# Whole 128x128 transposes with copies by parity, sinks ahead of transposes and reciprocals ahead of masks, in a banded attention on one core

## What is computed

```python
scores = scale * np.matmul(q, k.transpose(0, 1, 3, 2))
keep = is_sink | in_window
scores = np.where(keep, scores, -1000000000.0)
a = np.exp(scores - np.max(scores, axis=-1, keepdims=True))
a = a / (np.sum(a, axis=-1, keepdims=True) + 1e-09)
x = np.matmul(a, v)                       # heads side by side: 1536 x 512
x = np.maximum(x @ w_in, 0.0) ** 2 @ w_out          # 512 -> 2048 -> 512
h = x @ w2_in                                        # 512 -> 1024
solu = h * softmax(h)
out = (solu - mean) / sqrt(var + 1e-06) * g_ln @ w2_out
```

## Time and profile before

| | |
|---|---|
| median of 3 runs | 499.36 us (498.99 to 499.49) |
| profiled execution | 499.36 us, span of its profile 497.6 us |
| TensorE busy | 481.1 us, 97% of the span |
| VectorE, ScalarE, GpSimd busy | 58%, 50%, 21% |
| exponentials L480 | 46.7 us in 96 |
| scaling L402 | 45.7 us in 48 |
| DMA | 25.97 MB, nearly all in the first 130 us |

### The profile page before, as it was taken

How to read it: one execution, slowest core, us unless ns; L and a number is a source line. 1 busy time by engine, 2 the same in 40 slices (tenths; PEclk the granted TensorE clock), 3 DMA queues, 4 the chain that set the end, 5 groups by cost and what they waited for, 6 DMA issues and landing times.

```text
span 497.6 us, 7811 instructions
## 1 busy us (share of the span) xinstructions
PE 481.1 (97%) x2742; PEld 387.4 (78%) x2742; DVE 287.4 (58%) x678; ACT 248.0 (50%) x539; POOL 106.7 (21%) x129
## 2 busy tenths in 40 slices
PE   6889897999999999999999999999999999999997
PEld 3656575787888888888888888888888888888885
DVE  5788776368677454334435433444497666666651
ACT  3978878433443453344345334434356555545441
POOL 1876666049998000000000000000000000000000
PEclk9999999999999999999999999999999999999999
DMA  6768821170000000000000000000000000000001
GB/s 199 290 238 308 316 98 36 44 297 0 0 0 0 0 1 1 0 0 0 0 1 0 0 1 0 0 0 1 0 1 22 22 21 21 21 21 21 21 28 57
DMA packets 10138, 25.97 MB, mean 52 GB/s; under 512 B 3200, under 2 KB 5248, under 8 KB 8832
## 3 DMA queue, kind: packets, MB, share of 16 engines
q1 hardware_dynamic: 10112, 25.64, 14.1%
HBM read 22.48 MB, written 3.15 MB: 52 GB/s over the span
## 4 chain that ended last, share of the span: by engine, by line
PE 86%; ACT 6%; DVE 3%; DMA 3%; SPq 1%; POOL 1%; issue 1%; DVEq 0%
PE ps L1023 26%; PE ps L1038 26%; PE ps L1073 13%; PE ps L1052 13%; ACT probs L480 3%; PE ps L1059 2%; DMA k_sb<-in_k_t 2%; PE ps L951 2%; PE ps L906 1%; PE ps L915 1%; PE ps L961 1%; ACT pt_sb L488 1%; SPq L320 1%; POOL probs L402 1%; ACT x_hi L494 1%
## 5 line engine op out<-in xcount | busy, mean ns | idle before, releaser
L790 DVE CAST act_hi<-act_sq 128x512 fp32r<-128x512 f32 x48 | 26.0, 542 | 126.1 <-ACT act_sq L538 123.3
L533 ACT ACTIVATE ps<-ps 128x512 f32<-128x512 f32 x48 | 27.9, 582 | 141.4 <-PE ps L1023 141.4
L1023 PE MATMUL ps<-x_hi,w_in_hi 128*128 128x512 f32 x192 | 75.1, 391 | 0.0
L1038 PE MATMUL ps<-act_hi,w_out_hi 128*128 128x512 f32 x192 | 74.8, 390 | 0.1
L1023 PE MATMUL ps<-x_hi,w_in_lo 128*128 128x512 f32 x192 | 74.8, 389 | 0.0
L1023 PE MATMUL ps<-x_lo,w_in_hi 128*128 128x512 f32 x192 | 74.7, 389 | 0.0
L1038 PE MATMUL ps<-act_hi,w_out_lo 128*128 128x512 f32 x192 | 74.7, 389 | 0.0
L1038 PE MATMUL ps<-act_lo,w_out_hi 128*128 128x512 f32 x192 | 74.7, 389 | 0.0
L402 POOL TENSOR_TENSOR probs<-probs,row_inv 128x512 f32<-128x512 f32 (+1 forms) x48 | 45.7, 973 | 30.8 <-DVE row_inv L691 30.8
L480 ACT ACTIVATE probs<-probs,neg_max 128x272 f32<-128x272 f32 (+2 forms) x96 | 46.7, 497 | 7.1 <-DVE neg_max L678 7.0
L1023 PEld LDWEIGHTS ps<-x_hi,w_in_hi 128*128 128x128 f32 x192 | 36.0, 188 | 8.5 <-issue 1.2
(11 more groups left out here) (97 smaller groups left out, 829.3 us busy)
## 6 DMA issues: line engine op xcount, KB each, us to landing
w_in_raw<-in_w_in SPq DMA_DIRECT2D x4, 1024.0 KB, 4.8
w_out_raw<-in_w_out SPq DMA_DIRECT2D x4, 1024.0 KB, 8.2
k_sb<-in_k_t SPq DMA_DIRECT2D x8, 408.0 KB, 5.1
q_sb<-in_q_t SPq DMA_DIRECT2D x8, 384.0 KB, 4.2
v_sb<-in_v SPq DMA_DIRECT2D x16, 192.0 KB, 3.9
out<-out_sb SPq DMA_DIRECT2D x12, 256.0 KB, 2.0
w_in_raw<-in_w_in SPq DMA_DIRECT2D x1, 2048.0 KB, 9.4
w_out_raw<-in_w_out SPq DMA_DIRECT2D x1, 2048.0 KB, 13.8
```

Source lines behind the costliest of these rows:

```text
L533: nc.scalar.activation(ps[:, H_BANK + u, :], ps[:, H_BANK + u, :], ACT.Relu).then_inc(relu_done, 1)
L790: dve.tensor_copy(act_hi[:, u, :], act_sq[:, u, :]).then_inc(act_hi_done, 1)
L1023: last = mm(ps[:, H_BANK + u, :], w[:, u, c, :], x[:, c, t * TILE1:(t + 1) * TILE1], start=(c == 0 and m == 0), stop=(c == DC - 1 and m == 2))
L1038: last = mm(ps[:, Y_BANK + c, :], w[:, u, c * P:(c + 1) * P], a[:, u, :], start=(first and m == 0), stop=(final and m == 2), skip_group_ch ...
```

## The change

The numbered pieces of the diff: (1) each block is turned by one 128x128 transpose; a unit fills one bank, unit n bank 4 + n % 2. (2) ScalarE copies the even units, VectorE the odd ones; a unit waits for the copy of unit n-2 alone, and `weigh_key` for the copy of its own unit. (3) In step 0 of pair p keys 4, 5 and the sinks of pair p-1 stand ahead of the transposes. (4) The sinks take one 128-column matmul for both heads in place of two of 64 columns. (5) VectorE's `invert` stands ahead of `mask_group` in each step.

```diff
--- before.py
+++ after.py
@@ -188,15 +189,6 @@
     gen_ps = ps[:, S_BANK:S_BANK + 2, :].rearrange("p a b -> p (a b)")[:, 0:SEQ]
     gen_pt_ps = ps[:, PT_BANK:PT_BANK + 2, :].rearrange("p a b -> p (a b)")[:, 0:SEQ]
 
-    HQ = P // 2
-
-    def turned_part(m, h):
-
-        chunks = 8 if m < NG - 1 else 7
-        src = ps[:, PT_BANK + h, 0:HQ * chunks].rearrange("p (g q) -> p g q", q=HQ)
-        dst = pt_sb[:, :, :].rearrange("p n (g h q) -> p (n g) h q", g=4, h=2)[:, 8 * m:8 * m + chunks, h, :]
-        return dst, src
-
     def score_bank(g, u):
 
         return S_BANK + 2 * u + g % 2
...
@@ -481,11 +473,10 @@
                                                         bias=neg_max[:, b, u, i:i + 1], accum_out=row_sum[:, b, u, i:i + 1])
                 last.then_inc(exp_done, 1)
 
-            def copy_turned(p, m):
-
-                act.wait_ge(turned, NG * p + m + 1)
-                dst, src = turned_part(m, 0)
-                nc.scalar.activation(dst, src, ACT.Copy).then_inc(pt_low, 1)
+            def copy_turned(p, n):
+
+                act.wait_ge(turned, UNITS * p + n + 1)
+                nc.scalar.activation(pt_sb[:, n, :], ps[:, PT_BANK + n % 2, :], ACT.Copy).then_inc(pt_even, 1)
 
             def x_high(p):
 
...
@@ -500,7 +491,7 @@
                     for m in range(NG):
                         if m == 0 and p > 0:
                             x_high(p - 1)
-                        copy_turned(p, m)
+                        copy_turned(p, 2 * m)
                         if p < LAST:
                             exps(p + 1, m)
                     if p == 0:
...
@@ -690,11 +681,11 @@
                 dve.wait_ge(den_done, NG * p + k + 1)
                 dve.reciprocal(row_inv[:, b, :, blocks], row_den[:, b, :, blocks]).then_inc(inv_done, 1)
 
-            def copy_turned(p, m):
-
-                dve.wait_ge(turned, NG * p + m + 1)
-                dst, src = turned_part(m, 1)
-                dve.tensor_copy(dst, src).then_inc(pt_high, 1)
+            def copy_turned(p, n):
+
+                dve.wait_ge(turned, UNITS * p + n + 1)
+                width = 512 if n < QB - 1 else 3 * P
+                dve.tensor_copy(pt_sb[:, n, 0:width], ps[:, PT_BANK + n % 2, 0:width]).then_inc(pt_odd, 1)
 
             def x_low(p):
 
...
@@ -711,13 +702,13 @@
                 invert(0, 1)
                 for p in range(PAIRS):
                     for m in range(NG):
-                        if p < LAST:
-                            mask_group(p + 1, m)
                         if m == 0:
                             invert(p, 2)
                         elif p < LAST:
                             invert(p + 1, m - 1)
-                        copy_turned(p, m)
+                        if p < LAST:
+                            mask_group(p + 1, m)
+                        copy_turned(p, 2 * m + 1)
                         if m == 0 and p > 0:
                             x_low(p - 1)
                     if p == 0:
...
@@ -907,31 +898,25 @@
                                       keys[:, key:key + BAND_WIDTH[i]], start=True, stop=True)
                     last.then_inc(scores_done, 1)
 
-            def turn(n, g, columns):
-
-                for h in range(2):
-                    half = slice(HQ * h, HQ * (h + 1))
-                    at = 4 * HQ * (n % 2) + HQ * g
-                    last = nc.tensor.transpose(ps[:, PT_BANK + h, at:at + HQ], columns[half, :], identity[half, half])
-                return last
-
-            def turn_units(p, m):
-
-                b = p % 2
-                macro = NG * p + m
-                wait(pe, pt_low, macro)
-                wait(pe, pt_high, macro)
-                for n in (2 * m, 2 * m + 1):
-                    pe.wait_ge(probs_ready, (QB + 1) * p + min(n + 2, QB))
-                    for u in range(2):
-                        if n < QB - 1:
-                            turn(n, 2 * u, probs[:, b, u, own_at(n):own_at(n) + P])
-                            last = turn(n, 2 * u + 1, probs[:, b, u, prev_at(n + 1):prev_at(n + 1) + P])
-                        else:
-                            turn(n, u, probs[:, b, u, own_at(n):own_at(n) + P])
-                if m == NG - 1:
+            def turn(p, u, n, to, src):
+
+                at = to + (2 * P * u if n < QB - 1 else P * u)
+                return nc.tensor.transpose(ps[:, PT_BANK + n % 2, at:at + P], probs[:, p % 2, u, src:src + P], identity[:, :])
+
+            def turn_unit(p, n):
+
+                unit = UNITS * p + n
+                pe.wait_ge(probs_ready, (QB + 1) * p + min(n + 2, QB))
+                if unit >= 2:
+                    pe.wait_ge(pt_even if n % 2 == 0 else pt_odd, unit // 2)
+                for u in range(2):
+                    last = turn(p, u, n, 0, own_at(n))
+                    if n < QB - 1:
+                        last = turn(p, u, n, P, prev_at(n + 1))
+                if n == QB - 1:
                     pe.wait_ge(probs_ready, (QB + 1) * (p + 1))
-                    last = turn(QB - 1, 2, sink_probs[:, b, :, :, :].rearrange("p u i s -> p (u i s)"))
+                    sinks = sink_probs[:, p % 2, :, :, :].rearrange("p u i s -> p (u i s)")
+                    last = nc.tensor.transpose(ps[:, PT_BANK + n % 2, 2 * P:3 * P], sinks, identity[:, :])
                 last.then_inc(turned, 1)
 
             def weigh_key(p, j):
...
@@ -940,8 +925,7 @@
                 if j == 0:
                     pe.wait_ge(v_in[b], 16 * V_LOADS * (p // 2 + 1))
                     wait(pe, x_lo_done, 2 * p)
-                pe.wait_ge(pt_low, NG * p + j // 2 + 1)
-                pe.wait_ge(pt_high, NG * p + j // 2 + 1)
+                pe.wait_ge(pt_even if j % 2 == 0 else pt_odd, 3 * p + j // 2 + 1)
 
                 width = 2 * P if j < QB - 1 else P
                 cuts = [(0, P), (P, P)] if j == 2 else [(0, width)]
...
@@ -956,10 +940,8 @@
 
                 for i in range(2, QB):
                     col = P * i
-                    for u in range(2):
-                        rows = slice(HEAD_DIM * u, HEAD_DIM * (u + 1))
-                        last = mm(ps[rows, X_BANK + col // HALF, col % HALF:col % HALF + P], v_sinks[:, p % 2, i - 2, rows],
-                                  pt_sb[:, QB - 1, 2 * P:3 * P], start=False, stop=True, skip_group_check=True)
+                    last = mm(ps[:, X_BANK + col // HALF, col % HALF:col % HALF + P], v_sinks[:, p % 2, i - 2, :],
+                              pt_sb[:, QB - 1, 2 * P:3 * P], start=False, stop=True, skip_group_check=True)
                 last.then_inc(pv_done, 1)
 
             def banded_attention():
...
@@ -968,11 +950,12 @@
                 score_group(1, 0)
                 for p in range(PAIRS):
                     for m in range(NG):
-                        turn_units(p, m)
                         if m == 0 and p > 0:
                             weigh_key(p - 1, 4)
                             weigh_key(p - 1, 5)
                             weigh_sinks(p - 1)
+                        turn_unit(p, 2 * m)
+                        turn_unit(p, 2 * m + 1)
                         if m > 0:
                             weigh_key(p, 2 * m - 2)
                             weigh_key(p, 2 * m - 1)
```

More of the change, by code:

```diff
@@ L20 @@
 NP, NG = len(PIECES), len(GROUPS)
+UNITS = QB
 BAND_WIDTH = [P, 2 * P] + LATE * [BAND]
@@ L95, in build @@
     probs = att.take("probs", [P, 2, 2, ALL_BANDS])
-    pt_sb = att.take("pt_sb", [P, QB, 512])
+    pt_sb = att.take("pt_sb", [P, UNITS, 512])
     probs_end = att.at
@@ L226, in build @@
     turned = sem("turned")
-    pt_low = sem("pt_low_copied")
-    pt_high = sem("pt_high_copied")
+    pt_even = sem("pt_even_copied")
+    pt_odd = sem("pt_odd_copied")
     pv_done = sem("pv_done")
```

## The result

The changed kernel takes 505.12 us (median of 4 runs, 504.92 to 505.44), the kernel before 499.43 us beside it: the ratio is 1.0113, 95% interval 1.0101 to 1.0126. It is 5.7 us slower; forecast were 4.3 us, 503.7 in 501.2 to 506.9.

A forecast was written before the change was run, and what follows sets the result against it. A loop through ScalarE, VectorE, GpSimd and TensorE was taken to bound each attention pair. Middle pairs +2.1 us, first interval +0.5, pair 0 +1.0, last interval +0.7: together +4.3 on 499.36, so 503.7 us, range 501.2 to 506.9.

The forecast's parts named there:

- main term: Five middle pairs of the banded attention: 5 x 10.04 = 50.2 us against 48.06, +2.1.
- the ends: Attention before and after the five middle pairs: pair 0 +1.0 us, first interval +0.5, last interval +0.7.
- Part 4, the wait of VectorE: Sums and reciprocals ahead of the masks: VectorE waits for exponentials, and ScalarE idles 0.7 us, twice a pair.
- Part 2, transposes: Whole transposes on TensorE at 0.110 us a step: 23 blocks x 0.044 = 1.0 us more a pair.
- The new loop: One pair from x_hi through exponentials, reciprocal, masks, scores, transposes, values and sinks to the next x_hi: 10.04 us.
- The two are a tie: taking either cause away alone frees little.: Per pair, TensorE's queue without waits takes 9.97 us, the loop by way of VectorE 10.04; removing one cause frees little.
- TensorE's own round: TensorE's own queue over one pair, with no wait at all: 9.97 us.
- second rival: Gain of the earlier sinks cancels the rest: a pair 9.5 us, total 499.7; chance 0.07.
- Part 1: Sinks and values of pair p-1 ahead of pair p's transposes: up to 0.95 us a pair off ScalarE's wait of 1.33.
- The faster rival: ScalarE is freed before x_hi and the rest hides: a pair 8.8 us, total 495.8; chance 0.06.
- The k_sb waits: TensorE's two waits for k_sb in the middle pairs, 0.6 us each, vanish in the slower loop.
- Rival D: Waits for x_hi, masks and unit 5's copy add, or whole-shape changes cost 0.3: a pair 10.6 us, 507.5; chance 0.13.

The follow-up runs named there:

- e_split: The changed kernel with the sums and reciprocals of steps 1 and 2 between the masks of the group's first and second block; 499.96 us, ratio 1.0023.
- e_whole_sinks: The changed kernel with the reciprocals behind the masks again; 499.74 us, ratio 1.0011 to the kernel before.
- e_sinks_recip: The kernel before with keys 4, 5 and sinks ahead of the half transposes and reciprocals ahead of the masks; 506.26 us, ratio 1.0146.
- S: Keys 4, 5 and sinks of pair p-1 ahead of the transposes; alone on the kernel before 496.46 us, ratio 0.9942.
- e_sinks_wide: The kernel before with keys 4, 5 and sinks ahead of the half transposes, and sinks as 4 matmuls of 128 columns; 497.22 us.
- e_best: The kernel before with sinks ahead of the half transposes and VectorE's copy ahead of the reciprocals in steps 1 and 2; 496.34 us, repeated 495.80.

## Why the prediction was right, point by point

- **Direction and size.** Slower by 1.1%, inside the range and beside the point by 1.4 us: 5.7 measured, 4.3 forecast. The total is nearer than its main term, which was 2.0 too low: the ends were 0.3 too high and 0.5 came back unforeseen. That the errors offset is luck.
- **Part 4, the wait of VectorE.** Right in place, and to a few hundredths in size. From x_hi to the scores behind the first masks I had 4.26 us; the trace has 79.05 to 83.31, 4.26. ScalarE's two waits came as 0.66 and 0.59 (0.7 forecast), 9.4 us in all (10). e_split shows the cause.
- **Part 2, transposes.** Whole ones step by 0.11 us, as taken: 8 in 1.04 (78.85). Nine changes of shape at 0.15 fit for the transposes (74.21 to 75.13 is 0.92, as summed). For the sinks I had said "the same": they cost 0.21 more, 1.20 from their start to x_hi in place of 1.09, and 0.10 ahead of them, which I had counted.
- **The new loop, 10.04 for 10.48.** The step that failed is the term of scores 4, 5: 1.11 in the sum, 1.38 in the trace (72.83 to 74.21). I let the loop go through the mask of block 2 and forgot that block 5's scores wait for the mask of block 3, which comes 0.7 us later. The sinks' 0.11 and 0.05 in the values of keys 2, 3 make up the rest: 10.04 + 0.27 + 0.11 + 0.05 = 10.47.
- **"The two are a tie: taking either cause away alone frees little."** Wrong: the loop was 0.44 too short (10.04 for 10.48), and TensorE's own round 0.14 too long (9.97 for 9.83). Most of the 0.14 is a mistake of the sum: I closed the round at x_hi, but TensorE goes on 0.11 us before x_hi starts (74.48 and 74.59 in the earlier trace rows). With 10.48 against 9.83 there is no tie. Without the reciprocals the kernel loses its whole cost (e_whole_sinks). My second rival's time, 499.7, is what that kernel has, though not by its terms: a pair is 9.83 there and not 9.5. In the other direction it held: with the reciprocals first, half transposes gain nothing (e_sinks_recip).
- **Part 1.** The 0.95 us shows: the wait for x_hi fell from 1.33 to 0.83, and by itself S gives 2.9 us. The faster rival had 8.8 us a pair for this part alone; it is 8.91. What it needed beyond that, costless transposes and hidden reciprocals, was false.
- **The k_sb waits** vanished, as said, and did in every variant that isn't faster than the kernel before; in the faster ones one or both stay.
- **Sum.** Five middle intervals +4.1 (2.1 forecast; the difference is 4 x 0.44 and 0.25 for the fifth), pair 0 and the first interval +1.2 (1.5), the last +0.6 (0.7), and -0.5 behind it that I had not seen: the first chunks of the feed-forward waited for VectorE before and no longer do. Of the 1.5, 1.0 was for pair 0, which brought 0.5, and 0.5 for the first interval, which brought 0.7; its 10.61 rested on the wrong cut at 25.30.
- **Rival D** had a late copy of unit 5. It exists with half transposes (0.33 us a pair in e_sinks_recip). In the changed kernel the middle pairs don't have it, but the fifth interval does (0.66 at 87.78), which I had taken for a pair like the others.

## What to carry to other kernels

Where engines work in one ring, an operation that waits may stand ahead of others only if those are not needed before it can run; in front of the reciprocal the masks of one block were enough to hide its wait, and with none it cost 5 us. Follow such a loop through every wait of a group, not through its first instruction: the second mask was the missing 0.27 us of ten. And when a change is a bundle, run its parts crosswise: here one part was worth 2.9 us by itself, and 6.9 in the company of the two that cost.

## What the runs showed that I had not expected

- A change of the array's shape costs twice, 0.10 us in front and 0.05 to 0.11 in the first step behind. It does so into the whole shape too: in e_sinks_wide the first step of the sinks is 0.21 us and the others 0.11, and with the 0.10 in front that is 0.21 together. Between values and half transposes, eight sink matmuls of 64 columns are faster than four of 128 by just this much (0.22 us a pair).
- The granted clock can fall in one execution of a kernel and not in another: 0.57 over 3.6 us in e_best (a mix of 1.2 and 2.4 GHz), after TensorE had waited 1.25 us for masks at 27.1, and 1.00 in its repetition with the same wait. It cost 1.5 us, and read as an effect of the edit it misled me by one experiment.
